# First MLP's output with its columns on partitions, mean squares by a ones matmul and Newton steps, two PSUM banks for the hidden layer

## The chip, the cores and the metric

One core of a Trainium2 chip (trn2) runs the whole program. The metric is the device time of one execution in microseconds, and less is better. Matmuls run on TensorE (PE in the profile, its weight loads PEld), elementwise work on VectorE (DVE), ScalarE (ACT) and GpSimd (POOL), and SyncE (SP) issues the DMAs. PSUM, where matmuls write, has eight banks in each partition; they are `ps[:, 0, :]` to `ps[:, 7, :]` here.

## The reference

Attention over 4 batches of 8 heads, 576 positions and 64 columns feeds two MLPs. All is in float32.

```python
# attention: softmax over means of 4 positions (144 of them), repeated 4 times,
# plus softmax over the positions nearer than 4
x = attn_out.transpose(0, 2, 1, 3).reshape(2304, 512)
h = x @ w_in                        # 512 -> 2048
y = (h * np.cos(h)) @ w_out         # 2048 -> 512, the first MLP's output
rms = np.sqrt(np.mean(y * y, axis=-1, keepdims=True) + 1e-06)
yn = y / rms * rms_g
g, val = yn @ w_gate, yn @ w_val    # 512 -> 1536
out = (g / (1 + np.exp(-g)) * val) @ w_out2
```

## The kernel before

**Numbers.** Every float32 operand of a large matmul is split into a high part (rounded to the matmul's format, a copy on ScalarE) and a low part (the rest, a subtraction on VectorE or GpSimd). `three` then adds three matmuls: low by high, high by low, high by high.

**First MLP.** The 2304 tokens are worked off in six passes (chunks c = 0 to 5) of 384 tokens. A pass has 16 hidden tiles f of 128 columns. In step f TensorE issues `up(f)`, twelve matmuls of 384 columns into bank `HB[f % NH]`, and then `down(f - 3)`, which adds the finished tile f - 3 into y; steps 16 to 18 have downs only, the last pass ends after step 15. Between up and down ScalarE and VectorE turn the tile into h cos h: turns (ScalarE, L751), reduction to one turn (VectorE, L1053 and L1055), Abs and Sin (ScalarE, L757 and L759), product with the bank (VectorE, L1061, `g_done`), high part (ScalarE, L686) and low part (VectorE, L972). L1061 is the last to read the bank. The wait `g_done, F1 * c + max(f + 1, NH)` ahead of up(f) asks for the product of tile f - NH of the same pass, or, for the first NH tiles, for all of the pass before.

`down_tile` takes three tiles of 128 tokens (t): the hidden tile is the stationary operand, the weights stream with 512 columns, so y has its tokens on partitions, in three banks. At a pass's end ScalarE squares the three tiles with a sum along the row (`squares`), VectorE copies them to `XY` (`copy_y`), and GpSimd takes the power -0.5 and multiplies (`scale_y`).

**Attention in the passes.** Passes 0 to 2 hold the attention of the next batch, four pairs of heads each. The tables `PE_WHERE` and `BESIDE_WHERE` set behind which step's up or down TensorE, and behind which tile's operation ScalarE and VectorE, do a piece of it. For pair 0 TensorE does the scores of the first head in step 1 behind up(1), those of the second in steps 2 and 3, and the two groups of transposes in step 4; VectorE and ScalarE do their parts between the operations of tiles 0 to 4. These passes are a loop on each engine, `Fori(0, ACH)` with ACH = 3; passes 3 and 4 are a second loop, pass 5 is written out.

**Second MLP.** It works in three blocks of 768 tokens (two passes' y each), 12 steps a block, i = 0 to 35. Its operands have columns on partitions. For that TensorE transposes y, four 128 by 128 at a time (`turn`, L1350), six times a block: in steps 5 to 10 of pass 5 for the first block, in steps 1 to 6 of the block before for the others. VectorE multiplies them by the gain out of PSUM (`turn_out`, L1006), then forms four sums (`operand_sum`) and the low parts (`operand_low`). A step has seven products (a Strassen-like scheme, two pairs of 384 columns give gate and value) in the banks CA and CB, `filler` puts the six tiles of the second down, 512 columns each, between them. In step 0 it puts the last three downs of the first MLP there instead. ScalarE copies CA out between products (`snapshot`, L806), VectorE adds CB (L1096, L1101, L1106).

**Weights of the second MLP** are split in passes 3 to 5 by ScalarE (`weight_high`) and GpSimd (`weight_low`, L578) through three buffers wp and stored by SyncE.

Lines in rows are those of this kernel: L1274 to L1276 the three matmuls of `three`, L1350 the transposes, L1055 and L1061 two operations of a hidden tile.

## Time and profile before

| what | value |
|---|---|
| median of 3 runs | 998.36 us (997.68 to 998.68) |
| the profiled execution | 998.75 us, its span 996.6 us |
| TensorE busy | 960.0 us (96%) |
| VectorE, ScalarE, GpSimd busy | 576.2, 502.7, 313.9 us |
| mean granted clock of TensorE | 0.993 |

The span runs from the first to the last instruction of the profiled execution. In rows of the timeline the first number is the start in us from the span's start, the second the duration in us; "x3" counts merged instructions; in brackets stands how long the engine was idle before, and what ended that. Matmuls overlap, so the distance from one start to the next tells their price and not their duration. A first matmul of a group of up has the form `ps<-xs,W`, of down `ps<-W,ring`, of a product `ps<-xo,wu`.

The six passes of the first MLP begin at about 56, 156, 256, 356, 422 and 489 us, the second MLP at 554 us.

### The profile page before, as it was taken

The page shows a single profiled execution, that of the slowest core. Times are in us where ns is not written, and L with a number is a line of the kernel's source. Part 1 is how long each engine was busy: PE and PEld are TensorE (multiplying, and loading weights), DVE is VectorE, ACT ScalarE, POOL GpSimd, SP SyncE. Part 2 cuts the span into 40 slices and gives each one's busy share as a digit, 9 for nine tenths or more (in the row PEclk, how much of TensorE's full clock was granted, in tenths as well). Part 3 has the DMA queues.
Part 4 walks back from the last instruction along what each step waited for, and adds up shares of the span by engine and source line. Part 5 has one row for each costly group of instructions (what it writes and reads, how often), then busy time and mean ns, then how long its engine had stood idle before and what let it go on. Part 6 is the DMA issues. An engine that isn't in the chain of part 4 may idle for free.

```text
span 996.6 us, 17754 instructions
## 1 busy us (share of the span) xinstructions
PE 960.0 (96%) x6104; PEld 852.7 (86%) x6104; DVE 576.2 (58%) x1225; ACT 502.7 (50%) x1081; POOL 313.9 (32%) x366
## 2 busy tenths in 40 slices
PE   7899998999899999999999899999999999999998
PEld 6677787888788889899988788899899999999997
DVE  6767766766676665564557544455744445544434
ACT  4456665666566667676666533333522224423322
POOL 5937862321232146568486112111300001000000
PEclk9999999999999999999999899999999999999999
DMA  9522110211021025434344575555565455575531
GB/s 305 192 95 93 54 52 25 80 55 52 26 80 53 22 76 185 164 147 169 126 170 149 210 253 149 154 152 161 149 217 151 149 161 166 153 229 158 160 106 64
DMA packets 66176, 132.35 MB, mean 133 GB/s; under 512 B 7088, under 2 KB 7216, under 8 KB 66096
## 3 DMA queue, kind: packets, MB, share of 16 engines
q1 hardware_dynamic: 66096, 131.27, 41.4%
q8 instruction: 52, 0.85, 0.4%
q14 instruction: 28, 0.23, 0.1%
HBM read 104.50 MB, written 26.74 MB: 132 GB/s over the span
## 4 chain that ended last, share of the span: by engine, by line
PE 75%; DVE 9%; ACT 7%; issue 4%; POOL 4%; DMA 1%; DVEq 0%; ACTq 0%; POOLq 0%; SPq 0%
PE ps L1274 23%; PE ps L1276 23%; PE ps L1275 23%; DVE ub L1055 2%; DVE ub L1053 2%; ACT ub L757 2%; PE ps L1193 2%; POOL W L521 2%; PE ps L1210 1%; ACT ub L759 1%; PE ps L1350 1%; DVE XY L893 1%; ACT ub L751 1%; DVE ub L1061 1%; ACT probd L626 1%
## 5 line engine op out<-in xcount | busy, mean ns | idle before, releaser
L1274 PE MATMUL ps<-xo,wu 128*128 128x384 f32 x504 | 169.5, 336 | 5.2 <-ACT gate_a L806 3.7
L1275 PE MATMUL ps<-xo,wu 128*128 128x384 f32 x504 | 170.5, 338 | 0.0
L1276 PE MATMUL ps<-xo,wu 128*128 128x384 f32 x504 | 170.0, 337 | 0.0
L1274 PE MATMUL ps<-xs,W 128*128 128x384 f32 x384 | 136.0, 354 | 0.9 <-DVE xs L968 0.9
L1276 PE MATMUL ps<-xs,W 128*128 128x384 f32 x384 | 131.7, 343 | 4.8 <-issue 4.8
L1275 PE MATMUL ps<-xs,W 128*128 128x384 f32 x384 | 131.3, 342 | 0.0
L1274 PE MATMUL ps<-W,ring 128*128 128x512 f32 x288 | 116.5, 405 | 0.0
L1276 PE MATMUL ps<-W,ring 128*128 128x512 f32 x288 | 113.5, 394 | 0.0
L1275 PE MATMUL ps<-W,ring 128*128 128x512 f32 x288 | 113.4, 394 | 0.0
L1274 PEld LDWEIGHTS ps<-xo,wu 128*128 128x128 f32 x504 | 95.3, 189 | 12.4 <-ACT gate_a L806 4.1
L1275 PEld LDWEIGHTS ps<-xo,wu 128*128 128x128 f32 x504 | 95.1, 189 | 6.7
L1061 DVE TENSOR_TENSOR ub<-ub,ps 128x384 f32<-128x384 f32 x96 | 53.0, 552 | 73.6 <-ACT ub L759 73.6
L1276 PEld LDWEIGHTS ps<-xo,wu 128*128 128x128 f32 x504 | 95.2, 189 | 0.0
L757 ACT ACTIVATE ub<-ub 128x384 f32<-128x384 f32 x96 | 50.4, 525 | 72.1 <-DVE ub L1055 72.1
L1276 PE MATMUL ps<-wo,ring 128*128 128x512 f32 x216 | 85.7, 397 | 0.0
L1275 PE MATMUL ps<-wo,ring 128*128 128x512 f32 x216 | 85.4, 395 | 0.0
L1274 PE MATMUL ps<-wo,ring 128*128 128x512 f32 x216 | 85.3, 395 | 0.1
L1274 PEld LDWEIGHTS ps<-xs,W 128*128 128x128 f32 x384 | 74.0, 193 | 12.2 <-issue 7.7
L1101 DVE TENSOR_TENSOR val_b<-val_b,ps 128x384 f32<-128x384 f32 x36 | 19.9, 554 | 100.7 <-ACT val_b L806 100.5
L1275 PEld LDWEIGHTS ps<-xs,W 128*128 128x128 f32 x384 | 74.1, 193 | 1.8
L1053 DVE TENSOR_SCALAR ub<-ub 128x384 f32<-128x384 f32 x96 | 46.8, 488 | 49.1 <-ACT ub L751 49.0
L1276 PEld LDWEIGHTS ps<-xs,W 128*128 128x128 f32 x384 | 73.9, 192 | 0.0
(134 smaller groups left out, 1852.3 us busy)
## 6 DMA issues: line engine op xcount, KB each, us to landing
wu<-wsplit SPq DMA_DIRECT2D x252, 256.0 KB, 2.8
wsplit<-wp SPq DMA_DIRECT2D x84, 256.0 KB, 2.0
W_raw<-w SPq DMA_DIRECT2D x8, 1024.0 KB, 15.1
qk<-qk SPq DMA_DIRECT2D x14, 576.0 KB, 4.0
gv<-wgv SPq DMA_DIRECT2D x12, 512.0 KB, 3.6
vw<-vwin SPq DMA_DIRECT2D x14, 384.0 KB, 3.2
out<-XY SPq DMA_DIRECT2D x18, 256.0 KB, 3.4
vg<-vgrp SPq DMA_DIRECT2D x26, 144.0 KB
```

Of the source, the lines that this page charges most:

```text
L521: g.tensor_tensor(lo, raw, hi.bitcast(F32), ALU.subtract).then_inc(unit_ready, 1)
L626: ins = a.activation(kind.probd[j][0:QT, s, t, :], kind.sd[s][:, t * SD:t * SD + SD], ACT.Exp, scale=SCALE_D, bias=dbias[0:QT, s, t:t + 1] ...
L751: a.activation(v, HB[f % NH], ACT.Identity, scale=INV_2PI, bias=consts[:, 0:1]).then_inc(turns_ready, 1)
L757: a.activation(v, v, ACT.Abs).then_inc(abs_ready, 1)
L1053: v.tensor_scalar(w, w, MAGIC, -2.0 * math.pi, ALU.subtract, ALU.mult).then_inc(angle0, 1)
L1055: v.tensor_tensor(w, w, HB[f % NH], ALU.add).then_inc(angle_ready, 1)
L1061: v.tensor_tensor(w, w, HB[f % NH], ALU.mult).then_inc(g_done, 1)
L1101: v.tensor_tensor(vb[:, :], vb[:, :], CB, ALU.add).then_inc(vb_ready, 1)
L1193: ins = t_.matmul(sl[64 * half:64 * half + 64, t * WIN:t * WIN + WIN], q[:, Q0[w]:Q0[w] + WIN], k[:, K0[w]:K0[w] + WIN], start=False, stop ...
L1274: t_.matmul(dst, a_lo, b_hi, start=first, stop=False, skip_group_check=True)
L1275: t_.matmul(dst, a_hi, b_lo, start=False, stop=False, skip_group_check=True)
L1276: return t_.matmul(dst, a_hi, b_hi, start=False, stop=last, skip_group_check=True)
```

## The change

**Layout.** `down_tile(f, k)` now takes four tiles of 128 columns of y: the weights are the stationary operand, the hidden tile streams with its 384 tokens. y comes out with columns on partitions, in four banks (2 to 5). `turn` and `turn_out` are gone, and so are the copies xa and xb: the operands are read from XY.

**Mean squares.** They are now sums over partitions. ScalarE and VectorE copy two tiles of y each. GpSimd squares and adds the four (`squares`) and splits the sum in two parts; TensorE multiplies these by a matrix of ones (`stats`, two matmuls); VectorE computes the inverse root by a guess from the bits and three Newton steps (`rms_step`, steps 0 to 3) and scales the four parts by it and the gain (steps 4 to 7). For y of passes 0 to 3 this happens in the pass behind; for the last two in the second MLP.

**Banks.** The hidden tiles have two banks (NH = 2), CA is bank 0 and CB bank 6, which attention also uses.

**Other.** Operand sums and low parts of the first block move to tiles 5 to 13 of pass 5, and VectorE does all its low parts; XON = 9 slots hold the seven operands so that the first two of the next block don't wait. Six buffers wp instead of three. TensorE and VectorE have pass 0 written out and loop over passes 1 and 2.

```diff
+WPN = 6
+XON = 9
+NEWTON = 3
+RMS_STEPS = 1 + NEWTON + KT
+GUESS = float(0x5F3759DF)
+STAT = 6
...
+    xt = at("xt", [P, 3, 2, CH], F32, slots_at)
+    xo = at("xo", [P, XON, 2, 2, CH], F32R, slots_at + 2 * 4096 + 1024)
...
-    X, Z = ps[:, 3, :], ps[:, 7, :]
-
-    NH = 3
+    X, Z = ps[:, 6, :], ps[:, 7, :]
+
+    NH = 2
     HB = [ps[:, i, 0:CH] for i in range(NH)]
-    YB = [ps[:, 4 + i, :] for i in range(TT)]
-
-    CA, CB = ps[:, 1, 0:CH], ps[:, 2, 0:CH]
-    Y2 = [ps[:, i, :] for i in (3, 7, 0, 4, 5, 6)]
-
-    def turn_bank(c, t):
-        return ps[:, 2, :] if c else ps[:, (3, 7)[t % 2], :]
+    YB = [ps[:, 2 + k, 0:CH] for k in range(KT)]
+    STATS = X[:, 0:CH]
+
+    CA, CB = ps[:, 0, 0:CH], ps[:, 6, 0:CH]
+    Y2 = [ps[:, i, :] for i in (7, 1, 2, 3, 4, 5)]
 
...
-    POOL_XO = (1, 3, 5)
-    XO_ORDER = ((0, 1, 3, 2, 4, 5, 6), (0, 1, 2, 3, 4, 5, 6))
+    XO_ORDER = ((0, 1, 6, 3, 2, 4, 5), (0, 1, 2, 3, 4, 5, 6), (0, 1, 2, 3, 4, 5, 6))
+    POOL_XO = ((), (1, 3, 5), (1, 3, 5))
+    DVE_XO = ((0, 1, 6, 3, 2, 4, 5), (0, 2, 4, 6), (0, 2, 4, 6))
...
-    TURN_F = 1
-    TURN_STEP = 5
+    SUM_F = 7
+    STAT_AT = ((1, 2, 3, 4, 5, 6, 7, 8), (8, 9, 10, 12, 13, 14, 15, 16))
...
-            scale_y(b - 1)
-
...
+        def squares(c):
+
+            def square(k, to):
+                if k < 2:
+                    hold(pool, y_copied, 2 * c + k + 1)
+                else:
+                    hold(pool, y_copied_act, 2 * c + k - 1)
+                return g.tensor_tensor(sq[:, to, :], y_part(c, k), y_part(c, k), ALU.mult)
+
+            if not (isinstance(c, int) and c == 0):
+                hold(pool, newton, (2 + 3 * NEWTON) * c)
+            square(0, 0).then_inc(sq_ready, 1)
+            for k in range(1, KT):
+                square(k, 1).then_inc(sq_ready, 1)
+                hold(pool, sq_ready, (2 * KT - 1) * c + 2 * k)
+                g.tensor_tensor(sq[:, 0, :], sq[:, 0, :], sq[:, 1, :], ALU.add).then_inc(sq_ready, 1)
+                hold(pool, sq_ready, (2 * KT - 1) * c + 2 * k + 1)
+            if not (isinstance(c, int) and c == 0):
+                hold(pool, stat_done, c)
+            g.tensor_tensor(sums_of_sq[:, 0, :], sq[:, 0, :], ones[:, 0:1].to_broadcast([P, CH]), ALU.mult).then_inc(sshi_ready, 1)
+            hold(pool, sshi_ready, c + 1)
+            g.tensor_tensor(sums_of_sq[:, 1, :], sq[:, 0, :], sums_of_sq[:, 0, :].bitcast(F32), ALU.subtract).then_inc(sslo_ready, 1)
+            hold(pool, sslo_ready, c + 1)
 
         batch(1, (5, 5, 5, 1))
         with pool.Fori(2, B) as b:
+            squares(b - 2)
             batch(b)
+        squares(ACH - 1)
+
...
+            if f == 3:
+                squares(ACH)
+            elif f == 8:
+                squares(ACH + 1)
...
+            for o in {8: (0,), 9: (1,), 10: (6,), 11: (3,), 12: (2, 4), 13: (5,)}.get(f, ()):
...
-        def squares(c):
-
-            for t in range(TT):
-                if t == 0:
-                    act.wait_ge(down_done, F1 * c + F1)
-                    act.wait_ge(rinv_ready, c + 1)
-                    act.wait_ge(glo_ready, F1 * c + F1)
-                else:
-                    act.wait_ge(ssq_ready, TT * c + t)
-                junk = ub[:, :, :].rearrange("p a n -> p (a n)")[:, 0:512]
-                a.activation(junk, YB[t], ACT.Square, accum_out=ssq[:, t:t + 1]).then_inc(ssq_ready, 1)
-            act.wait_ge(ssq_ready, TT * c + TT)
+        def copy_y(c):
+
+            act.wait_ge(down_done, F1 * c + F1)
+            for k in range(2, KT):
+                a.activation(y_part(c, k), YB[k], ACT.Copy).then_inc(y_copied_act, 1)
 
...
+        def rms_step(c, step, at_=STATS):
+
+            x, y, r = sq[:, 0, :], sq[:, 1, :], rms[:, :]
+            n = (2 + 3 * NEWTON) * c
+            if step == 0:
+                dve.wait_ge(stat_done, c + 1)
+                v.tensor_scalar(x, at_, 1.0 / DM, 1e-6, ALU.mult, ALU.add).then_inc(ms_ready, 1)
+                dve.wait_ge(ms_ready, c + 1)
+                v.tensor_scalar(r.bitcast(I32), x.bitcast(I32), -0.5, GUESS, ALU.mult, ALU.add).then_inc(newton, 1)
+                dve.wait_ge(newton, n + 1)
+                v.tensor_scalar(x, x, -0.5, None, ALU.mult).then_inc(newton, 1)
+            elif step <= NEWTON:
+                n += 2 + 3 * (step - 1)
+                dve.wait_ge(newton, n)
+                v.tensor_tensor(y, r, r, ALU.mult).then_inc(newton, 1)
+                dve.wait_ge(newton, n + 1)
+                v.tensor_tensor(y, y, x, ALU.mult).then_inc(newton, 1)
+                dve.wait_ge(newton, n + 2)
+                ins = v.scalar_tensor_tensor(r, y, 1.5, r, ALU.add, ALU.mult).then_inc(newton, 1)
+            else:
+                k = step - NEWTON - 1
+                if k == 0:
+                    dve.wait_ge(newton, n + 2 + 3 * NEWTON)
+                    dve.wait_ge(g_in, 16)
+                v.scalar_tensor_tensor(y_part(c, k), y_part(c, k), gcol[:, k:k + 1], r, ALU.mult, ALU.mult).then_inc(y_scaled, 1)
+
+        def operand_sum(c, step):
...
+            if 5 <= f <= 8:
+                operand_sum(0, f - 5)
+            for o in {9: (0,), 10: (1,), 11: (6,), 12: (3, 2), 13: (4, 5)}.get(f, ()):
+                operand_low(0, o)
...
+                if before and attention and f == 2:
+                    rms_step(c - 1, 0)
                 if attention:
                     attend(c, f, 1)
+                if before and not last and STAT + attention < f <= STAT + RMS_STEPS:
+                    rms_step(c - 1, f - STAT - 1)
...
-        with dve.Fori(0, ACH) as c:
+        hidden(0, True)
+        split_x(1)
+        copy_y(0)
...
+            for n, at_ in enumerate(STAT_AT):
+                if i in at_[1:]:
+                    rms_step(LASTC - 1 + n, at_.index(i))
...
+            if kind is Narrow and j == 0 and s == 0 and not (isinstance(b, int) and b == 1):
+                pe.wait_ge(ms_ready, b - 1)
...
-        def down_tile(f, t):
-            cols = slice(t * P, t * P + P)
+        def down_tile(f, k):
+            cols = slice(k * P, k * P + P)
             slot = 2 * f + 1
-            return three(YB[t], ring[:, f % 3, 0, cols], ring[:, f % 3, 1, cols], w_part(slot, 0), w_part(slot, 1), f == 0, f == F1 - 1)
+            return three(YB[k], w_part(slot, 0)[:, cols], w_part(slot, 1)[:, cols], ring[:, f % 3, 0, :], ring[:, f % 3, 1, :], f == 0, f == F1 - 1)
 
         def down(f):
-            for t in range(TT):
-                ins = down_tile(f, t)
+            for k in range(KT):
+                ins = down_tile(f, k)
             return ins
+
+        def stats(c, dst):
+
+            pe.wait_ge(sslo_ready, c + 1)
+            t_.matmul(dst, ones_r[:, :], sums_of_sq[:, 1, :], start=True, stop=False, skip_group_check=True)
+            t_.matmul(dst, ones_r[:, :], sums_of_sq[:, 0, :], start=False, stop=True, skip_group_check=True).then_inc(stat_done, 1)
 
         def attend(b, step, half):
 
...
-                        pe.wait_ge(y_copied, TT * c + TT)
+                    if f == 0 and before:
+                        pe.wait_ge(y_copied, 2 * c)
+                        pe.wait_ge(y_copied_act, 2 * c)
                     down(f).then_inc(down_done, 1)
-                if last and TURN_STEP <= step < TURN_STEP + PT6:
-                    turn(0, step - TURN_STEP)
+                if before and attention and step == 3:
+                    pe.wait_ge(diff_ready, 2 * PAIRS * (c + 1) + 2)
+                    stats(c - 1, STATS)
+                elif before and not attention and not last and step == STAT:
+                    stats(c - 1, STATS)
                 if attention:
                     attend(c + 1, step, 1)
...
-        with pe.Fori(0, ACH) as c:
+        chunk1(0, True)
+        with pe.Fori(1, ACH) as c:
             chunk1(c, True)
         with pe.Fori(ACH, LASTC) as c:
             chunk1(c, False)
-
-        def turn(c, t):
-
-            pe.wait_ge(y_scaled, PT6 * c + t + 1)
-            if c:
-                pe.wait_ge(gb_ready, F2 * (c - 1) + TURN_F + t + 1)
-            elif t >= 2:
-                pe.wait_ge(turned, t - 1)
-            bank, y = turn_bank(c, t), y2_tile(c, t)
-            for k in range(KT):
-                ins = t_.transpose(bank[:, k * P:k * P + P], y[:, k * P:k * P + P], ident[:, :])
-            ins.then_inc(tr_done, 1)
 
         def product(i, o, dst, first):
...
-                for n in ((0, 1), (2,), (3, 4), (5, 6), (7, 8))[slot]:
+                for n in ((0, 1, 2), (3,), (4, 5, 6), (7, 8, 9), (10, 11))[slot]:
...
-                pe.wait_ge(g_done, F1 * LASTC + F1 - 2 + NH)
+                pe.wait_ge(g_done, F1 * LASTC + F1 - 1 + NH)
             product(i, 0, CA, True)
             if i:
                 pe.wait_ge(gb_ready, i)
-            else:
-                pe.wait_ge(g_done, F1 * LASTC + F1 - 1 + NH)
-            if c < SC - 1 and TURN_F < f <= TURN_F + PT6:
-                pe.wait_ge(turned, PT6 * (c + 1) + f - TURN_F)
+            for n, at_ in enumerate(STAT_AT):
+                if i == at_[0] + 1:
+                    pe.wait_ge(ms_ready, LASTC + n)
...
-            if c < SC - 1 and TURN_F <= f < TURN_F + PT6:
-                turn(c + 1, f - TURN_F)
+            for n, at_ in enumerate(STAT_AT):
+                if i == at_[0]:
+                    pe.wait_ge(gb_ready, i + 1)
+                    stats(LASTC - 1 + n, CB)
```

TensorE, step 1 of the second MLP, around the place behind product 6 (`wo` with `ring_133` or `ring_134` is the second down). Before:

```order
L1276 MATMUL ps<-xo,wu_128 128x384
L1274 MATMUL ps<-wo,ring_133 128x512
L1275 MATMUL ps<-wo,ring_133 128x512
L1276 MATMUL ps<-wo,ring_133 128x512
L1350 MATMUL ps<-ident,XY 128x128 x4
L1274 MATMUL ps<-wo,ring_133 128x512
```

Now:

```order
L1306 MATMUL ps<-xo,wu_129 128x384
L1304 MATMUL ps<-wo,ring_134 128x512
L1305 MATMUL ps<-wo,ring_134 128x512
L1306 MATMUL ps<-wo,ring_134 128x512
L1330 MATMUL ps<-sums_of_sq,ones_r 128x384
L1331 MATMUL ps<-sums_of_sq,ones_r 128x384
L1304 MATMUL ps<-wo,ring_134 128x512
```

The four transposes are gone here and in steps 2 to 6; two ones matmuls stand in step 1 and again in step 8.

VectorE, attention passes, tile 2 and the copy of the transposed probabilities behind it. Before:

```order
L1053 TENSOR_SCALAR ub<-ub 128x384
L1055 TENSOR_TENSOR ub<-ub,ps 128x384
L972 TENSOR_TENSOR ring<-ub,ring 128x384
L1061 TENSOR_TENSOR ub<-ub,ps 128x384
L1052 REGISTER_ALU
```

Now, in passes 1 and 2:

```order
L1070 TENSOR_SCALAR ub<-ub 128x384
L1072 TENSOR_TENSOR ub<-ub,ps 128x384
L982 TENSOR_TENSOR ring<-ub,ring 128x384
L1078 TENSOR_TENSOR ub<-ub,ps 128x384
L1009 TENSOR_SCALAR sq<-ps 128x384
L1011 TENSOR_SCALAR rms<-sq 128x384
L1012 ISA
L1013 TENSOR_SCALAR sq<-sq 128x384
L953 COPY probd_85<-ps 72x288
```

The first step of the inverse root comes between the product of tile 2 and what follows it.

VectorE, pass 5 of the first MLP, from what stands behind tile 13 to the start of tile 15 (each tile begins with the reduction of `ub`). Before:

```order
L1020 TENSOR_TENSOR xb<-xb 128x768
L1023 TENSOR_TENSOR xt<-xa,xt 128x768
L1053 TENSOR_SCALAR ub<-ub 128x384
L1055 TENSOR_TENSOR ub<-ub,ps 128x384
L972 TENSOR_TENSOR ring<-ub,ring 128x384
L1061 TENSOR_TENSOR ub<-ub,ps 128x384
L1028 TENSOR_TENSOR xo<-xt,xo 128x768
L1028 TENSOR_TENSOR xo<-xb,xo 128x768
L1053 TENSOR_SCALAR ub<-ub 128x384
```

Now:

```order
L1052 TENSOR_TENSOR xo<-XY,xo 128x768
L1052 TENSOR_TENSOR xo<-xt,xo 128x768
L1070 TENSOR_SCALAR ub<-ub 128x384
L1072 TENSOR_TENSOR ub<-ub,ps 128x384
L982 TENSOR_TENSOR ring<-ub,ring 128x384
L1078 TENSOR_TENSOR ub<-ub,ps 128x384
L1070 TENSOR_SCALAR ub<-ub 128x384
```

The sums that stood behind tile 13 come earlier now, the low parts that stood behind tile 14 stand behind tile 13 at the latest, and between tiles 14 and 15 VectorE does nothing else.

## Rows read from the trace of the kernel before

**Rows 1.** The page, part 4: the chain that ended last, by engine.
```profile
PE 75%; DVE 9%; ACT 7%; issue 4%; POOL 4%; DMA 1%; DVEq 0%; ACTq 0%; POOLq 0%; SPq 0%
```

**Rows 2.** Busy time: stretch, length, each engine's busy us, clock, DMA.
```profile
157.00:257.00 100.00, 95.51 (x800) 80.53 (x800) 66.70 (x175) 62.69 (x136) 25.62 (x37) 0.98 0.17 53
356.00:422.00 66.00, 66.00 (x334) 59.92 (x333) 37.06 (x71) 46.12 (x103) 40.86 (x50) 1.00 0.40 146
```

**Rows 3.** Timeline: start, duration, instruction; TensorE and VectorE, start of pass 4.
```profile
426.61 0.33 PE L1274 MATMUL ps<-xs,W 128*128 128x384 f32 x1
...
427.69 0.56 DVE L1061 TENSOR_TENSOR ub<-ub,ps 128x384 f32<-128x384 f32 x1 [1.24 <-ACT ub L759]
...
428.69 0.33 PE L1274 MATMUL ps<-xs,W 128*128 128x384 f32 x1
...
430.96 0.55 DVE L1061 TENSOR_TENSOR ub<-ub,ps 128x384 f32<-128x384 f32 x1 [0.77 <-ACT ub L759]
...
432.85 0.33 PE L1274 MATMUL ps<-xs,W 128*128 128x384 f32 x1
```

**Rows 4.** Timeline, TensorE and VectorE, in attention pass 1.
```profile
159.30 0.33 PE L1276 MATMUL ps<-xs,W 128*128 128x384 f32 x1 [2.57 <-issue]
...
166.34 0.45 PE L1274 MATMUL ps<-xs,W 128*128 128x384 f32 x1
...
167.72 0.54 DVE L1061 TENSOR_TENSOR ub<-ub,ps 128x384 f32<-128x384 f32 x1
...
169.51 0.44 PE L1274 MATMUL ps<-xs,W 128*128 128x384 f32 x1
...
175.43 0.33 PE L1274 MATMUL ps<-xs,W 128*128 128x384 f32 x1
...
179.73 0.56 DVE L1061 TENSOR_TENSOR ub<-ub,ps 128x384 f32<-128x384 f32 x1 [2.05 <-ACT ub L759]
...
181.37 0.42 PE L1274 MATMUL ps<-xs,W 128*128 128x384 f32 x1
...
200.56 0.42 PE L1274 MATMUL ps<-xs,W 128*128 128x384 f32 x1
...
201.51 0.55 DVE L1061 TENSOR_TENSOR ub<-ub,ps 128x384 f32<-128x384 f32 x1 [2.05 <-ACT ub L759]
```

**Rows 5.** Busy time of two stretches; the granted clock is the 0.50.
```profile
161.00:164.00 3.00, 3.00 (x11) 3.00 (x11) 1.41 (x2) 0.89 (x2) 2.73 (x4) 0.50 0.03 5
560.20:566.80 6.60, 5.07 (x15) 4.88 (x16) 2.99 (x5) 3.82 (x6) 0.00 (x0) 0.50 0.01 2
```

**Rows 6.** Timeline: TensorE's first matmul of steps 6, 7 and 8, second MLP.
```profile
635.56 0.34 PE L1274 MATMUL ps<-xo,wu 128*128 128x384 f32 x1
...
647.82 0.34 PE L1274 MATMUL ps<-xo,wu 128*128 128x384 f32 x1
...
659.34 0.33 PE L1274 MATMUL ps<-xo,wu 128*128 128x384 f32 x1
```

**Rows 7.** Timeline, TensorE, in pass 5 of the first MLP.
```profile
503.82 0.33 PE L1274 MATMUL ps<-xs,W 128*128 128x384 f32 x1
...
523.75 0.30 PE L1350 MATMUL ps<-ident,XY 128*128 128x128 f32 x1 [1.71 <-DVE xa L1006]
...
533.37 0.42 PE L1274 MATMUL ps<-xs,W 128*128 128x384 f32 x1
```

**Rows 8.** Timeline, TensorE, from the first MLP's end into the second.
```profile
550.18 0.33 PE L1274 MATMUL ps<-xs,W 128*128 128x384 f32 x1
...
561.73 0.69 PE L1274 MATMUL ps<-xo,wu 128*128 128x384 f32 x1 [3.71 <-ACT gate_a L806]
...
574.26 0.33 PE L1274 MATMUL ps<-xo,wu 128*128 128x384 f32 x1
```

**Rows 9.** Groups of instructions: line, shapes, count, busy and mean, idle ahead.
```profile
L1101 DVE TENSOR_TENSOR val_b<-val_b,ps 128x384 f32<-128x384 f32 x36 | 19.9, 554 | 100.7 <-ACT val_b L806 100.5
...
L578 POOL TENSOR_TENSOR wp<-gv,wp 128x256 fp32r<-128x256 f32 x48 | 39.0, 813 | 32.3 <-ACT wp L722 29.6
```

243 lines of the change are left out of this document (99 added, 144 removed).

## The prediction

> **What bounds the kernel now.** First I read the chain that ended last, on the profile's page [rows 1]: TensorE carries 75% of it, VectorE 9%, ScalarE 7%. Then the busy time of two stretches [rows 2]. In a layer pass without attention TensorE is busy 66.00 of 66 us; in one with attention 95.5 of 100, VectorE 67, ScalarE 63, GpSimd 26. So whatever TensorE no longer issues is time won, and whatever makes it wait for VectorE or ScalarE is time lost. VectorE and ScalarE work as one serial chain per hidden tile f: turns (L751), reduction (L1053, L1055), Abs, Sin, product (L1061). I call the product's end *free(f)*: from then on the bank of HB that up(f) filled may be written again. The sum below is made against the profiled execution, 998.75 us (span 996.6 and 2.1 around it); the median of the runs is 998.36.
>
> **Two banks instead of three.** With NH = 3, up(f) waits for free(f-3); with NH = 2 for free(f-2). Where up(f+2) starts before free(f) today, the new wait costs at least the difference. In the pass that begins at 422 us [rows 3], up(2) starts at 426.61 and free(0) is 427.69 + 0.56 = 428.25; up(3) starts at 428.69 and free(1) is 430.96 + 0.55 = 431.51. Up(2) waits 1.6 us; behind its own 2.08 us up(3) waits again until free(1), 2.8 after its start today. ScalarE no longer squares y there, which brings this forward by some 0.2: 2.6 a pass. Nothing stands behind the waiting matmuls that could fill in, since the first down comes in step 3; down(0) and all later work move back. Later in a pass up and down together take 4.16 us a step [rows 3], the chain has two of these for a tile, and I count nothing. Passes 3, 4 and 5: 2.3 + 2.6 + 2.6 = +7.5.
>
> In the attention passes VectorE and ScalarE put softmax work of the next batch between two tiles. In pass 1 [rows 4] up(2) starts at 166.34, free(0) is 168.26; worse, up(4) starts at 175.43 and free(2) is 179.73 + 0.56 = 180.29. These 12.0 us from free(0) to free(2) belong to ScalarE and VectorE (two softmax halves and a table load), so TensorE can't shorten them; that it delivers local and downsampled scores later adds an estimated 0.4. Shift at up(4): 4.9 + 0.4 = 5.3; in passes 0 and 2 I read the same. +15.9 for three. Lower end: 4.9 each, 14.7.
>
> Right behind it stands a dependency that three banks hid: ScalarE and VectorE, after free(2), copy the first transposed probabilities, which TensorE makes behind up(4). Today up(4) is long done by then; now both engines wait until up(4) and seven transposes have run (some 3.7 us), then need 0.5 for the copy and some 3.4 for tile 3 (free(1) follows free(0) by 3.3 in rows 3), so free(3) is about 7.6 after up(4) starts, while TensorE would reach up(5) after 5.9 (its pitch today, 175.43 to 181.37 [rows 4]). +1.6 a pass, between 0 and 2.5: +4.8. In step 6 the same figure as at f=2 recurs smaller [rows 4]: up(8) starts at 200.56, free(6) is 202.06; +1.5 a pass, +4.5.
>
> **The clock.** After 2.57 us of idle at 156.7 [rows 4] the granted clock was 0.50 in 161 to 164 [rows 5]; after 3.71 us before 561.73 [rows 8] it was 0.50 from 560.2 to 566.8. Half clock for 3.4 us costs 1.7, for 6.6 us 3.3, less what falls into idle time (about a third in the second case). The new idle before up(4) is about 4 us long, in each attention pass. I take 2.2 each, +6.6; bounds 0 and 3.3 each. In the other three passes the idle comes in two pieces of 1.6 and 1 us, both shorter than the shortest above that was followed by half clock: 0, upper end 1.7 each.
>
> **The loop over the attention passes begins at 1.** TensorE's program now has pass 0 written out, so the jump back happens once, not twice. At the jump to pass 1 it idles for 2.57 us with "issue" as the reason [rows 4] and then has the half-clock stretch [rows 5], together 2.57 + 1.8 = 4.4. Taken as gone: -4.4. Bounds: the straight code may be fetched late as well (0), or all goes.
>
> **Transposes out.** Steps of the second MLP with four transposes take 647.82 - 635.56 = 12.26 us, without 659.34 - 647.82 = 11.52 [rows 6]; twelve such steps, 0.75 each: -9.0. In the last pass of the first MLP six more: from 503.82 to 533.37 six steps take 29.55 instead of 6 x 4.16 = 25.0, one with 1.71 of idle [rows 7]: -4.6. VectorE's multiplications out of the turned banks go too; they lay beside matmuls.
>
> **The ones matmuls.** Six pairs at 384 columns, by up's twelve in 2.08 us 0.17 each, 0.35 a pair. Two lie in passes 1 and 2 within the new idle time, four count: +1.4. They wait for GpSimd: 9 operations of 384 columns a pass, of which the row for 256 columns shows 0.81 us [rows 9]; by columns 1.2 each, 11 us behind the copy of y, between 7 and 15. They are asked for in step 3 of an attention pass (over 15 us after its start) and step 6 otherwise (over 21): hidden. GpSimd's own queue behind it is value sums and the splitting of gate and value weights; six wp buffers instead of three let ScalarE run ahead meanwhile.
>
> **Newton steps.** On VectorE each is three operations that wait for each other, 0.55 apiece by the nearest row, 1.7 a step. In the second MLP VectorE is idle 100.7 us in 36 steps ahead of L1101, 2.8 a step [rows 9]: hidden. In passes 3 and 4 the chain grows to some 4.6 us a step for four steps, 1.7 in all against about 2.7 of lead: hidden. In passes 1 and 2 the second falls directly ahead of L1053 of tile 10, right behind a softmax: between 0 and 1.7, I take 1.1: +2.2.
>
> **Down in four tiles.** Up and down take 4.16 a step, so nine matmuls of 512 columns take 2.08 [rows 3], just what twelve of 384 take in up: 0, between -1 and +2 in all 96.
>
> **The handover to the second MLP.** Up(15) starts at 550.18, product 2 of step 0 at 561.73 after 3.71 us of idle, at half clock; step 1 begins at 574.26, 24.1 us after up(15) [rows 8]. The operand sums and low parts are moved from steps 11 to 14 into 5 to 13, so tiles 14 and 15 run clean: I get free(15) at 7 us after up(15) starts, the snapshot at 8.1, with TensorE there at 7.9. Then up(15) and down(12) 4.2, the seven products 7.4 (11.52 less six tiles of 0.69) and twelve down tiles 6.3, with 0.4 of waits: 18.3. -5.8; bounds -2.3 (still waits, half clock stays) and -6.3.
>
> **Sum.** 7.5 + 15.9 + 4.8 + 4.5 + 6.6 + 1.4 + 2.2 = 42.9 lost; 4.4 + 9.0 + 4.6 + 5.8 = 23.8 won; +19.1. Some of TensorE's own small waits in the attention passes (about 2 us each) should shrink when it runs later; I take 2 off for all: +17, 1016 us against 998.75.
>
> A page of the Trainium skill speaks for the other side: TensorE: Matmul & The Clock Gate, "HAM oscillation — how this bites in real kernels", reports a kernel in which doubling PSUM buffers on top of a good loop order gave no further gain, that is, bank depth need not matter. By that rule the 32.7 us that hang on the bank, and the clock behind it, would be nothing. The rows agree with it only for the steady steps of a pass; at its start they don't.
>
> **Rivals.** *Two banks are enough* (faster): if VectorE and ScalarE caught up because their own work shrinks at a pass's start (no squares, fewer copies), the bank terms and the clock (39.3) vanish, 998.4 - 23.8 + 3.6 gives 978. Against it: 12 us between free(0) and free(2) hold no square and no copy of y. It decides from free(2) coming before 176. *The waits are there but alone*: no coupling behind up(4), no half clock, Newton hidden, TensorE's own waits shrink more: 19.1 - 4.8 - 6.6 - 2.2 - 3 = +3, 1001 to 1005. For it: every term is read from starts in a schedule that will shift. *The clock takes more*: half clock for 6.6 us in all three attention passes and 3.4 in the others, and the handover keeps its idle: 3.3 + 5.1 + 3.5 more, 1028. *The change doesn't reach the chip's order*: the wait counts are formed from NH everywhere, so no chance worth a number.
>
> **Numbers.** Forecast 0.65 (1008 to 1024), two banks enough 0.09, the waits alone 0.15, the clock takes more 0.11. The range reaches from 1001 to 1029. What this measurement can tell from no change is about 0.2%, 2 us: faster 0.09, within it 0.04 (the lower edge of the waits alone), slower 0.87.
>
> **What would show it.** In the profile after: idle of TensorE that ends on VectorE's product ahead of up matmuls, 1.6 and 1 us at the start of passes 3 to 5, about 4 us before the fifth up of passes 0 to 2; half clock behind the latter; no idle with "issue" at the first pass's end; second MLP steps of 11.5 us throughout, and step 0 near 14 instead of 19.9. If the first three passes are not longer than 100 us each, the forecast is wrong in its main term; if step 0 is still near 20, in the handover.

## The result and the profile after

| kernel | median of its runs | range |
|---|---|---|
| before | 998.02 us (4 runs) | 996.59 to 998.68 |
| after | 1034.89 us (4 runs) | 1033.68 to 1037.66 |

The ratio is 1.0375 (95% interval 1.0350 to 1.0399): 3.75% slower. The forecast was 1016 with a range of 1001 to 1029. It had the sign, and the time lies 6 us above the range. The profiled execution of after has a span of 1032.7 us against 996.6, so 36.1 us are to be explained where 17 were forecast.

Part 1 of the page of after:

```profile
PE 961.7 (93%) x6332; PEld 889.6 (86%) x6332; DVE 630.7 (61%) x1300; ACT 495.9 (48%) x1057; POOL 336.4 (33%) x385
```

TensorE is as busy as before (960.0) and stands still 34 us longer; VectorE has 54.5 us more work. The chain that ended last, which answers to [rows 1]:

```profile
PE 70%; DVE 13%; ACT 7%; POOL 5%; issue 4%; DMA 0%; POOLq 0%; ACTq 0%; DVEq 0%; SPq 0%
```

VectorE's share of the chain went from 9% to 13%. The groups of instructions say what TensorE waits for (behind the bar: busy time, mean ns, idle before and its releaser):

```profile
L1304 PE MATMUL ps<-xs,W 128*128 128x384 f32 x384 | 139.3, 363 | 48.1 <-DVE ub L1078 46.6
```

46.6 us in front of an up matmul end on VectorE's product L1078, the instruction that frees a bank; before, the same matmuls waited 0.9. Busy time by pass of after, as in [rows 2]:

```profile
165.00:274.00 109.00, 97.48 (x855) 88.21 (x854) 75.94 (x192) 62.48 (x134) 29.51 (x41) 0.98 0.16 49
381.00:456.00 75.00, 69.05 (x390) 67.03 (x389) 52.58 (x86) 44.73 (x99) 44.70 (x53) 1.00 0.36 131
```

In pass 3 VectorE was busy for 37.06 of 66 us and is now for 52.58 of 75. To see where the time went I take the distance between the first up matmuls of neighbouring passes, in us; the last column runs from the first product to the end.

| kernel | pass 0 | 1 | 2 | 3 | 4 | 5 | second MLP |
|---|---|---|---|---|---|---|---|
| before | 102.0 | 100.2 | 99.3 | 66.8 | 66.8 | 65.2 | 442.3 |
| after | 109.9 | 108.4 | 108.0 | 74.6 | 76.5 | 71.7 | 428.3 |
| difference | +7.9 | +8.2 | +8.6 | +7.8 | +9.7 | +6.5 | -14.0 |

With 1.3 us more ahead of pass 0 that is the 36 us. The terms of the prediction, sorted by pass, give about 27.6 for passes 0 to 2, 2.7, 3.0 and -2.0 for passes 3, 4 and 5, and -14.1 for the second MLP. The attention passes together came out within 3 us of the forecast and the second MLP within 0.1 us, and **the miss is in passes 3 to 5: 24.0 instead of 3.6.** That the attention passes fit is in part luck: two errors of opposite sign meet there, as the part on the prediction shows.

What was foreseen is there. At the start of pass 3 up(2) and up(3) wait, in attention pass 1 up(4) and up(5) do; these timelines of TensorE answer to [rows 3] and [rows 4]:

```profile
388.01 0.45 PE L1304 MATMUL ps<-xs,W 128*128 128x384 f32 x1 [2.04 <-DVE ub L1078]
...
390.90 0.44 PE L1304 MATMUL ps<-xs,W 128*128 128x384 f32 x1 [0.51 <-DVE ub L1078]
```

```profile
172.64 0.44 PE L1304 MATMUL ps<-xs,W 128*128 128x384 f32 x1 [1.50 <-DVE ub L1078]
...
184.94 0.68 PE L1304 MATMUL ps<-xs,W 128*128 128x384 f32 x1 [3.49 <-DVE ub L1078]
...
185.74 0.52 PE L1306 MATMUL ps<-xs,W 128*128 128x384 f32 x1
...
193.28 0.44 PE L1304 MATMUL ps<-xs,W 128*128 128x384 f32 x1 [1.10 <-DVE ub L1078]
```

Durations of 0.52 instead of 0.33 behind 184.94 are half clock. Windows of 3.4 to 3.7 us that begin at the end of three waits (columns as in [rows 2]; the clock is the third number from the end):

```profile
65.60:69.00 3.40, 3.40 (x11) 3.40 (x12) 1.69 (x4) 3.00 (x5) 0.00 (x0) 0.51 0.00 0
184.90:188.30 3.40, 3.36 (x11) 3.36 (x12) 1.52 (x3) 0.00 (x0) 1.92 (x3) 0.51 0.02 7
193.30:197.00 3.70, 3.70 (x60) 3.25 (x60) 3.33 (x6) 1.75 (x4) 0.00 (x0) 1.00 0.00 0
```

Half clock followed waits of 1.60 and 3.49 us, not the one of 1.10. The first products of steps 0, 1, 2 and 3 of the second MLP, in answer to [rows 6] and [rows 8], are 13.66, 12.14 and 11.53 us apart; the forecast was 14 and 11.5, against 19.9 for step 0 before. Step 1, with two ones matmuls, takes 0.6 more than a step without:

```profile
604.38 0.44 PE L1304 MATMUL ps<-xo,wu 128*128 128x384 f32 x1
...
618.04 0.33 PE L1304 MATMUL ps<-xo,wu 128*128 128x384 f32 x1
...
630.18 0.34 PE L1304 MATMUL ps<-xo,wu 128*128 128x384 f32 x1
...
641.71 0.33 PE L1304 MATMUL ps<-xo,wu 128*128 128x384 f32 x1
```

Two things were not foreseen. **Late in passes 3 and 4** up(12) and up(13) wait:

```profile
430.29 0.45 PE L1304 MATMUL ps<-xs,W 128*128 128x384 f32 x1 [1.32 <-DVE ub L1078]
...
435.99 0.44 PE L1304 MATMUL ps<-xs,W 128*128 128x384 f32 x1 [1.26 <-DVE ub L1078]
```

VectorE shows why. Here is its timeline for one tile, from one L1078 (the product that frees the bank) to the next:

```profile
417.74 0.55 DVE L1078 TENSOR_TENSOR ub<-ub,ps 128x384 f32<-128x384 f32 x1 [0.77 <-ACT ub L779]
418.21 1.10 DVE L1017 TENSOR_TENSOR sq<-rms 128x384 f32<-128x384 f32 x1
419.35 0.97 DVE L1019 TENSOR_TENSOR sq<-sq 128x384 f32<-128x384 f32 x1
420.36 0.98 DVE L1021 SCALAR_TENSOR_TENSOR rms<-sq,rms 128x384 f32<-128x384 f32 x1
421.26 0.35 DVE L1070 TENSOR_SCALAR ub<-ub 128x384 f32<-128x384 f32 x1
421.65 0.56 DVE L1072 TENSOR_TENSOR ub<-ub,ps 128x384 f32<-128x384 f32 x1
422.12 0.55 DVE L982 TENSOR_TENSOR ring<-ub,ring 128x384 fp32r<-128x384 f32 x1
423.44 0.55 DVE L1078 TENSOR_TENSOR ub<-ub,ps 128x384 f32<-128x384 f32 x1 [0.78 <-ACT ub L779]
```

The tile takes 5.70 us, TensorE's up and down 4.16; the products of tiles 9, 10 and 11 come 5.70, 6.24 and 5.70 us behind the one before. The Newton step in it (L1017 to L1021) takes 3.05 us, not the 1.7 of the prediction. The next rows, of pass 4, show on what that depends; those of GpSimd in the same time stand below them:

```profile
500.62 1.11 DVE L1017 TENSOR_TENSOR sq<-rms 128x384 f32<-128x384 f32 x1
501.76 0.98 DVE L1019 TENSOR_TENSOR sq<-sq 128x384 f32<-128x384 f32 x1
502.77 0.56 DVE L1021 SCALAR_TENSOR_TENSOR rms<-sq,rms 128x384 f32<-128x384 f32 x1
```

```profile
500.56 0.75 POOL L609 TENSOR_TENSOR wp_more<-gvs,wp_more 128x256 fp32r<-128x256 f32 x1 [2.94 <-ACT wp_more L751]
501.39 0.93 POOL L609 TENSOR_TENSOR wp_more<-gv,wp_more 128x256 fp32r<-128x256 f32 x1
```

GpSimd ends at 502.32. The operation that begins after that takes 0.56, those beside it 1.0 to 1.1. The ones with an operand in PSUM (L1078, L1072) take 0.55 either way. L1021 at 502.77 and the L1070 and L982 of the tile above, without an operand in PSUM, take their short time because GpSimd is idle then. **In pass 5** up(6) stands still for 5.64 us and runs at half clock behind it. ScalarE had stood still ahead of it, for GpSimd's sums:

```profile
552.60 0.42 ACT L751 ACTIVATE wp<-gvs 128x256 fp32r<-128x256 f32 x1 [5.06 <-POOL gvs L595]
555.83 0.42 ACT L751 ACTIVATE wp<-gvs 128x256 fp32r<-128x256 f32 x1 [2.82 <-POOL gvs L599]
556.16 0.56 ACT L771 ACTIVATE ub<-ps,consts 128x384 f32<-128x384 f32 x1
```

L771 forms the turns of the next tile, its first operation. GpSimd's queue in the same time, its last squares and the first sum behind them:

```profile
548.70 1.00 POOL L575 TENSOR_TENSOR sq<-sq 128x384 f32<-128x384 f32 x1
549.78 0.83 POOL L579 TENSOR_TENSOR sums_of_sq<-sq,ones 128x384 fp32r<-128x384 f32 x1
550.68 1.01 POOL L581 TENSOR_TENSOR sums_of_sq<-sq,sums_of_sq 128x384 fp32r<-128x384 f32 x1
551.77 0.73 POOL L595 TENSOR_TENSOR gvs<-gv 128x256 f32<-128x256 f32 x1
```

### The profile page after: what moved, and what is told of

It is laid out like the page before. It is cut to its first block, busy times and chain, and to the rows that moved or that the text cites. A ratio compares the mean times of both kernels' runs of the same rounds, so it can differ in the third digit from the quotient of the medians.

```text
span 1032.7 us, 18242 instructions
## 1 busy us (share of the span) xinstructions
PE 961.7 (93%) x6332; PEld 889.6 (86%) x6332; DVE 630.7 (61%) x1300; ACT 495.9 (48%) x1057; POOL 336.4 (33%) x385
## 4 chain that ended last, share of the span: by engine, by line
PE 70%; DVE 13%; ACT 7%; POOL 5%; issue 4%; DMA 0%; POOLq 0%; ACTq 0%; DVEq 0%; SPq 0%
PE ps L1304 22%; PE ps L1306 21%; PE ps L1305 21%; DVE ub L1070 3%; DVE ub L1072 2%; ACT ub L779 2%; ACT ub L777 2%; PE ps L1221 2%; POOL W L538 1%; DVE ub L1078 1%; PE ps L1238 1%; PE ps L1281 1%; DVE sq L1019 1%; DVE sq L1017 1%; ACT L779 1%
## 5 line engine op out<-in xcount | busy, mean ns | idle before, releaser
L1304 PE MATMUL ps<-xs,W 128*128 128x384 f32 x384 | 139.3, 363 | 48.1 <-DVE ub L1078 46.6
L1306 PE MATMUL ps<-xs,W 128*128 128x384 f32 x384 | 133.6, 348 | 0.0
L1305 PE MATMUL ps<-xs,W 128*128 128x384 f32 x384 | 133.3, 347 | 0.0
L1304 PE MATMUL ps<-ring,W 128*128 128x384 f32 x384 | 132.4, 345 | 0.8 <-DVE ring L982 0.8
L1306 PE MATMUL ps<-ring,W 128*128 128x384 f32 x384 | 128.7, 335 | 0.0
L1305 PE MATMUL ps<-ring,W 128*128 128x384 f32 x384 | 128.5, 335 | 0.0
L1304 PEld LDWEIGHTS ps<-xs,W 128*128 128x128 f32 x384 | 75.4, 196 | 59.2 <-DVE ub L1078 34.7
L1078 DVE TENSOR_TENSOR ub<-ub,ps 128x384 f32<-128x384 f32 x96 | 53.0, 552 | 74.1 <-ACT ub L779 74.1
L1070 DVE TENSOR_SCALAR ub<-ub 128x384 f32<-128x384 f32 x96 | 55.5, 579 | 37.2 <-ACT ub L771 37.2
L1304 PEld LDWEIGHTS ps<-ring,W 128*128 128x128 f32 x384 | 72.3, 188 | 4.8 <-issue 4.1
L1305 PEld LDWEIGHTS ps<-xs,W 128*128 128x128 f32 x384 | 75.9, 198 | 0.0
L1306 PEld LDWEIGHTS ps<-xs,W 128*128 128x128 f32 x384 | 75.7, 197 | 0.0
```

The source lines that it names most:

```text
L1070: v.tensor_scalar(w, w, MAGIC, -2.0 * math.pi, ALU.subtract, ALU.mult).then_inc(angle0, 1)
L1078: v.tensor_tensor(w, w, HB[f % NH], ALU.mult).then_inc(g_done, 1)
L1304: t_.matmul(dst, a_lo, b_hi, start=first, stop=False, skip_group_check=True)
L1305: t_.matmul(dst, a_hi, b_lo, start=False, stop=False, skip_group_check=True)
L1306: return t_.matmul(dst, a_hi, b_hi, start=False, stop=last, skip_group_check=True)
```

## Experiments

Each kernel is held against before by its ratio on the same chip; after has 1.0375. Spans and pass times are those of one profiled execution each. Before itself had medians of 998.0, 995.1, 997.0 and 996.1 us on the chips used, so a difference of spans can be off by some 3 us, and the ratio decides on the total. "Not told apart" below means that the 95% intervals of two ratios overlap. Narrow stands for Newton operations on 8 columns.

**1. Before with two banks.** The handover's waits follow the banks. All else stays: down in three tiles of 512 columns, the transposes and the squares on ScalarE.

```diff
-    NH = 3
+    NH = 2
-    CA, CB = ps[:, 1, 0:CH], ps[:, 2, 0:CH]
-    Y2 = [ps[:, i, :] for i in (3, 7, 0, 4, 5, 6)]
+    CA, CB = ps[:, 0, 0:CH], ps[:, 2, 0:CH]
+    Y2 = [ps[:, i, :] for i in (3, 7, 1, 4, 5, 6)]
```

> The kernel before with NH = 2 alone (CA in bank 0 and one output tile in bank 1, so that the handover stays legal); layout, transposes, squares and weights as before. Theory (the second waits on the bank are the largest part of the loss): passes 0 to 2 grow by 7 to 9 us each, clock included, passes 3 to 5 by 2.3 to 2.8 each, together +28 to +34, about 1029 us. TensorE idles 3.5 to 4 us ahead of the fifth up of passes 0 to 2. Rival (the new work on VectorE and GpSimd is what makes the engines late, the bank only passes it on): under +10.

Measured: ratio 1.0309 (1.0291 to 1.0328), which is 30.8 us. Passes 111.6, 107.9, 107.4, 69.5, 69.8, 66.7, that is +9.7, +7.7, +8.1, +2.7, +3.0, +1.6. The theory holds, with passes 0 and 4 above its ranges and pass 5 below. The waits at the start of pass 3 and before up(4) and up(5) of pass 1 are close to those of after:

```profile
388.74 0.44 PE L1274 MATMUL ps<-xs,W 128*128 128x384 f32 x1 [1.66 <-DVE ub L1061]
```

```profile
191.05 0.69 PE L1274 MATMUL ps<-xs,W 128*128 128x384 f32 x1 [3.86 <-DVE ub L1061]
...
200.21 0.44 PE L1274 MATMUL ps<-xs,W 128*128 128x384 f32 x1 [0.68 <-DVE ub L1061]
```

Two banks alone cost about 3.1%. In the attention passes of this profile that is 25.5 us; after has 24.7 there, with Newton's cost and the loop's gain in it. The 25.5 may be some us too high: the profiled execution took 1031.6 us, 5.0 above the median of its runs, and its span grew by 33.2 where the ratio says 30.8. In passes 3 to 5 it is 7.3 us (forecast 7.5) of after's 24.0, and 16.7 are left.

**2. Before with pass 0 of the attention passes written out,** so that TensorE loops over passes 1 and 2 as in after.

```diff
-        with pe.Fori(0, ACH) as c:
+        chunk1(0, True)
+        with pe.Fori(1, ACH) as c:
             chunk1(c, True)
```

> The kernel before, TensorE's loop over attention passes from 1, pass 0 written out, nothing else. Theory (the idle with reason issue is the jump back): the 2.57 us of idle and the half clock behind it at the first pass's end go, -3.5 to -4.5 us, about 994. Rival (the idle is caused by something else at a pass's start, such as the copy of y): no change, 998.

Measured: ratio 0.9961 (0.9947 to 0.9975), passes 0 to 2 100.2, 96.7, 96.9. By the ratio that is 3.9 us less; the theory holds in the total. Yet both stretches of idle time that nothing released are gone, that between passes 1 and 2 too, although a jump back stands there still, and pass 0, which has no turn ahead of it, shows 1.7 less too. The up group that had 4.8 us of it:

```profile
L1276 PE MATMUL ps<-xs,W 128*128 128x384 f32 x384 | 130.0, 339 | 0.0
```

**3. Before with all three attention passes written out.**

```diff
-        with pe.Fori(0, ACH) as c:
+        for c in range(ACH):
             chunk1(c, True)
```

> The before kernel with TensorE's three attention passes written out one after the other instead of as a loop of three. With only pass 0 written out the ratio was 0.9961 (0.9947 to 0.9975) and both stretches of idle time that nothing released (2.57 and 2.26 us) were gone, the second one too although a loop of two with a jump back stayed. Theory (the idle time goes with a long loop body whose code comes back from far, and is gone as soon as the loop is short of one turn): the same as with pass 0 alone, 0.9950 to 0.9972. Rival (the jump back still costs something that the profile shows in another row, such as the wait of 1.7 us for the exponents at the start of passes 1 and 2): 0.990 to 0.994.

Measured: ratio 0.9969 (0.9957 to 0.9981), the same as pass 0 alone. The theory holds; the second jump costs nothing that can be measured. Either is faster than both kernels of this case.

**4. After with GpSimd's squares of the fourth panel (y of pass 4) behind the last of the second MLP's twelve weight tiles** instead of behind the ninth. The f of this piece of GpSimd's program counts weight tiles, not hidden tiles; in the trace the squares begin at 587.15 instead of in front of up(6).

```diff
-            elif f == 8:
+            elif f == F2 - 1:
                 squares(ACH + 1)
```

> The changed kernel, GpSimd's squares of y of pass 4 moved behind the last weight (from behind f = 8). Theory (in pass 5 ScalarE waits 5.1 and 2.8 us for gate sums that stand behind the squares in GpSimd's queue, the product of tile 4 is late, up(6) idles 5.6 us and the clock falls): pass 5 shrinks from 71.7 to 64 to 66 us, total -6 to -8, about 1028. Rival (ScalarE would wait for free wp buffers or stores anyway): -2 at most.

Measured: ratio 1.0374 (1.0354 to 1.0393), no gain in the time where the theory had 6 to 8 us. Pass 5 took 67.5 instead of 71.7 us (theory 64 to 66); its up(6) is now without a wait, and up(15) has a new one:

```profile
559.95 0.33 PE L1304 MATMUL ps<-xs,W 128*128 128x384 f32 x1
...
596.10 0.41 PE L1304 MATMUL ps<-xs,W 128*128 128x384 f32 x1 [1.88 <-DVE ub L1078]
```

So the cause of the 5.64 us is shown, and moving it is worth 4.2 in its pass. In this profile passes 2 and 3 took 1.4 and 0.8 us more, with half clock in other places; the span fell by 2.8, the median relative to before not at all. The gain is seen in its pass and is not shown in the total.

**5. After with the Newton steps of passes 3 and 4 on a PSUM operand** (y in the free bank Z), so that two of the three operations have one input in PSUM, with GpSimd as busy as ever.

```diff
-            x, y, r = sq[:, 0, :], sq[:, 1, :], rms[:, :]
+            x, y, r = sq[:, 0, :], sq[:, 1, :] if y is None else y, rms[:, :]
...
-                    rms_step(c - 1, f - STAT - 1)
+                    rms_step(c - 1, f - STAT - 1, y=None if attention else Z[:, 0:CH])
```

> The changed kernel, in passes 3 and 4 the Newton steps' intermediate y lies in PSUM bank 7, which is free there, instead of SBUF. Theory (VectorE operations with two SBUF inputs take 1.1 instead of 0.55 us while GpSimd works): the second and third operation of a Newton step fall from 0.98 to 0.55 us in those passes, the first stays at 1.09; passes 3 and 4 shrink by 1.5 to 2.5 us each, -3 to -5 in all. Rival (the operations are long because they wait for each other's results): durations and time stay.

Measured: ratio 1.0363 (1.0339 to 1.0388); passes 3 and 4 72.8 and 74.1, 1.8 and 2.4 less, within the theory's 1.5 to 2.5 each. Passes 1 and 2 of this profile took 0.3 and 1.0 more, and the total is not told apart from after's. The same step in its timeline of VectorE:

```profile
419.71 0.56 DVE L1078 TENSOR_TENSOR ub<-ub,ps 128x384 f32<-128x384 f32 x1 [0.77 <-ACT ub L779]
420.18 1.11 DVE L1017 TENSOR_TENSOR ps<-rms 128x384 f32<-128x384 f32 x1
421.32 0.57 DVE L1019 TENSOR_TENSOR ps<-ps,sq 128x384 f32<-128x384 f32 x1
421.93 0.56 DVE L1021 SCALAR_TENSOR_TENSOR rms<-ps,rms 128x384 f32<-128x384 f32 x1
...
424.74 0.56 DVE L1078 TENSOR_TENSOR ub<-ub,ps 128x384 f32<-128x384 f32 x1 [0.77 <-ACT ub L779]
```

Only L1017, whose two inputs are still in SBUF, takes 1.11; the other two fell from 0.98 to 0.57 and the tile from 5.70 to 5.03 us. That shows the contention with GpSimd as the cause of the long operations.

**6. After with the Newton operations on 8 of 384 columns.** The other 376 columns keep the starting value of the inverse root, so the kernel leaves their Newton steps out.

```diff
             elif step <= NEWTON:
+                x, y, r = sq[:, 0, 0:8], sq[:, 1, 0:8], rms[:, 0:8]
```

> The changed kernel with VectorE's two operations of each Newton step on 8 of the 384 columns: the inverse root is left at its starting value for the other columns, all else is as in the changed kernel. It takes away VectorE's time for the steps (3.05 us for one step in passes 3 and 4) and keeps their place and number. Theory (the steps make VectorE's work for a tile 5.7 us where TensorE's is 4.16, three tiles in a row in each pass that has them): the idle stretches before up(12) and up(13) of passes 1 to 4 go, and the late down behind; 2 to 3 us from each of passes 1 and 2, 4 to 5 from passes 3 and 4; in all 12 to 15 us less, a ratio to before of 1.023 to 1.026. Rival (what is late there is the chain of the mean squares, or GpSimd's sums, and not VectorE's time): under 5 us less, as with the steps on a PSUM operand, ratio 1.033 or more.

Measured: ratio 1.0268 (1.0231 to 1.0305), span 1020.9, 11.8 less (10.7 by the ratio). Passes 1 to 4 took 105.8, 105.4, 70.8, 72.9: 2.6, 2.5, 3.8 and 3.5 less, and the waits before up(12) and up(13) are gone. The mechanism of the theory holds; its sizes were too high: 12 to 15 us in all and 4 to 5 in passes 3 and 4 each. The tile is now 4.10 us:

```profile
417.61 0.56 DVE L1079 TENSOR_TENSOR ub<-ub,ps 128x384 f32<-128x384 f32 x1 [0.78 <-ACT ub L779]
418.08 0.70 DVE L1018 TENSOR_TENSOR sq<-rms 128x8 f32<-128x8 f32 x1
418.81 0.17 DVE L1020 TENSOR_TENSOR sq<-sq 128x8 f32<-128x8 f32 x1
419.01 0.59 DVE L1022 SCALAR_TENSOR_TENSOR rms<-sq,rms 128x8 f32<-128x8 f32 x1
...
421.71 0.56 DVE L1079 TENSOR_TENSOR ub<-ub,ps 128x384 f32<-128x384 f32 x1 [0.77 <-ACT ub L779]
```

**7. After with three banks in passes 3 to 5.**

```diff
+    HB3 = [Z[:, 0:CH], HB[0], HB[1]]
+    def hb(f, attention):
+        return HB[f % NH] if attention else HB3[f % 3]
...
-                    pe.wait_ge(g_done, F1 * c + max(f + 1, NH))
+                    pe.wait_ge(g_done, F1 * c + max(f + attention, NH))
```

> The changed kernel with three banks for the inner layer again in passes 3 to 5 (the bank that holds Z or the mean squares in the attention passes is free there), two banks in passes 0 to 2. The before kernel with two banks took 2.7, 3.0 and 1.6 us more in passes 3 to 5 than before; the changed one 7.8, 9.7 and 6.5 more. Theory (a third bank is one step of 4.16 us of slack for whatever makes the end of a tile late: the Newton steps on VectorE and the sums on GpSimd): the idle stretches before up(2) and up(3) go, those before up(12) and up(13) of passes 3 and 4 (1.3 us each in the records, and the late down behind them) shrink to near nothing, the 5.6 us before up(6) of pass 5 to about 1.5; passes 3, 4 and 5 take 68 to 70, 68 to 70 and 67 to 68 us instead of 74.6, 76.5 and 71.7; in all 15 to 20 us less than the changed kernel, a ratio to before of 1.018 to 1.023. Rival (the third bank pays only for the waits at the start of each pass, and the engines behind are late whatever the banks): 7.3 us less, ratio 1.030.

Measured: ratio 1.0369 (1.0343 to 1.0396). Passes 3 to 5 73.1, 76.2, 68.5, second MLP 433.0. My theory fell, and the rival too. The waits at the start of the passes are gone and those before up(12) and up(13) as well; the one before up(6) of pass 5 is now one of 5.13 before a down. In pass 3 waits come back before the downs:

```profile
445.99 0.41 PE L1309 MATMUL ps<-ring,W 128*128 128x384 f32 x1 [1.86 <-DVE ring L987]
...
450.18 0.41 PE L1309 MATMUL ps<-ring,W 128*128 128x384 f32 x1 [1.87 <-DVE ring L987]
```

A third bank lets one late tile pass. It doesn't help where VectorE needs more time per tile than TensorE over several tiles and has too little to spare before the pass ends. What pass 5 gains the second MLP loses: its step 0 takes 4.7 us more (2.97 of idle for ScalarE's snapshot, and half clock), as it does, by 6, in experiments 8, 10 and 11. VectorE's product of tile 15 ends 74.3 us after the start of pass 5 in after and 74.3 here. TensorE is through with its ups sooner and then waits for the same product and the snapshot behind it. From the start of pass 5 to the end of the kernel it is 501.5 us here and 500.0 in after.

**8. Three banks and narrow Newton steps together** (the edits of 7 and 6).

> The changed kernel with three banks in passes 3 to 5 and with VectorE's two operations of each Newton step on 8 of the 384 columns (the inverse root stays at its starting value for the others). The three banks alone brought nothing in the sum: passes 3, 4, 5 took 73.1, 76.2, 68.5 us instead of 74.6, 76.5, 71.7 while the second MLP took 4.7 us more, and the idle time moved from the ups to the downs at the end of passes 3 and 4. The narrow steps alone made passes 3 and 4 70.8 and 72.9. Theory (VectorE has more work than TensorE over tiles 11 to 15, and a bank only puts off when that shows; with the work gone the bank is worth what it is in the before kernel, 2.7 to 3.0 us a pass): passes 3 and 4 at 67 to 68 and 68.5 to 70 us; ratio to before 1.019 to 1.023 (narrow steps alone 1.0268). Rival (the third bank is worth nothing here whatever VectorE does, since the sums of squares on GpSimd and the longer VectorE operations beside them set the starts): passes 3 and 4 at 70 and 72 or more, ratio 1.026 or more.

Measured: ratio 1.0219 (1.0196 to 1.0243), passes 3 and 4 67.2 and 69.7. The theory holds, the rival (1.026 or more) doesn't: once VectorE keeps up, the third bank is worth 3.7 and 3.2 us a pass.

**9. After with the first transposes of pass 0 ahead of up(4).**

```diff
+    PE_WHERE0 = (((1, 0), (2, 0), (3, 0), (3, 1), (4, 1), (5, 0)),) + PE_WHERE[1:]
-            for what, j in steps_at(PE_STEPS, PE_WHERE, (step, half)):
+            for what, j in steps_at(PE_STEPS, PE_WHERE0 if isinstance(b, int) and b == 1 else PE_WHERE, (step, half)):
```

> The changed kernel with TensorE's transposes of the first head of a pair, in pass 0 only, ahead of up(4) instead of behind it. Theory (with two banks up(4) waits 3.9 us for VectorE's last operation on tile 2, the transposes stand behind it in TensorE's queue, and what copies them and the next tile's end come late for that: the 2.0 us before up(5)): the wait before up(4) stays near 3.9, that before up(5) falls from 2.0 to under 0.7, pass 0 takes 1.3 to 2 us less, ratio 1.0355 to 1.036. Rival (up(5) waits for the second bank alone, and what is behind it is slack): within 0.5 us of the changed kernel, ratio 1.037 to 1.0375; or the copies that now come earlier push VectorE's last operation on tile 2 back, and up(4) waits longer: 1 us more, 1.0385.

Measured: ratio 1.0355 (1.0330 to 1.0379), pass 0 107.5, 2.4 less, and no wait before up(5). So the coupling is real: the copies, and with them the next tile, wait for the transposes that stand behind up(4). The total is not told apart from after's; pass 2 of this profile took 3.3 more, with half clock there.

**10. Three banks, late squares and early transposes.**

> The changed kernel with three edits together: three banks in passes 3 to 5, GpSimd's squares of the fourth panel behind the last tile of pass 5 instead of behind tile 8, and the early transposes in pass 0. Theory (each takes its own wait): passes 3 to 5 at 68 to 70, 68 to 70 and 65 to 66 us, pass 0 1.5 us shorter; 17 to 24 us less than the changed kernel, ratio 1.014 to 1.020; still slower than before, since the two banks in the attention passes stay (the before kernel with two banks took 9.7, 7.7 and 8.1 us more in these). Rival (the edits pay for the same waits): no more than the three banks alone, within 1 us.

Measured: ratio 1.0282 (1.0256 to 1.0308), span 1023.4: 9.3 us less than after, not 17 to 24, since passes 3 and 4 stayed at 73.2 and 74.6 and the second MLP took 434.3. Pass 5 took 62.2: with both edits the waits before its ups are gone and one of 1.56 before a down is left, where either edit alone left 67.5 or more. But from the start of pass 5 to the end the kernel takes 496.4 us, and 495.7 with the late squares alone: behind tile 15 the third bank gives nothing.

**11. All four edits** (10 and the narrow steps).

> The changed kernel with all four: three banks in passes 3 to 5, the narrow Newton steps (inverse root left at its starting value in 376 of 384 columns), GpSimd's squares of the fourth panel behind pass 5, and the early transposes in pass 0. It is the closure of the account: what is left should be the two banks of the attention passes (7.7 to 9.7 us a pass by the before kernel with two banks, less what the early transposes and the loop from 1 give) and the second MLP's gain. Theory: pass 0 105 to 106, passes 1 and 2 105 to 107 each, pass 3 67 to 68, pass 4 68.5 to 70, pass 5 62 to 63, second MLP 432 to 435; span 1003 to 1008, ratio 1.008 to 1.014. Rival (the edits overlap and there is a cost not yet named in passes 3 to 5): span 1013 or more, ratio 1.018 or more.

Measured: span 1003.8, ratio 1.0148 (1.0125 to 1.0171). Passes 104.4, 105.8, 105.4, 67.2, 69.7, 62.1, second MLP 434.4. The span and all stretches but pass 0 (0.6 below) are in the theory's ranges, the ratio is 0.0008 above its own. This profiled execution was the fastest of its four, 4.1 us below their median, at a clock of 0.992 against 0.986 to 0.990, so its pass times may flatter the kernel by up to as much. Within that the account closes: what is left against before in passes 3 to 5 is 0.3 us, in the attention passes 14.2, in the second MLP -7.9 instead of -14.0. The 6 us between these last two are pass 5's lateness, which the third bank moves into step 0.

## Why the prediction was wrong

**The step that failed is "Newton steps", where it says of passes 3 and 4: "the chain grows to some 4.6 us a step for four steps, 1.7 in all against about 2.7 of lead: hidden."** Each operation was priced at 0.55 us by the nearest row. The row shown is L1101 [rows 9], which has an operand in PSUM and stands in the second MLP, where GpSimd is idle. In passes 3 and 4 GpSimd works beside the Newton operations, and they take 0.97 to 1.11. The products of three tiles come 5.70, 6.24 and 5.70 us apart, not 4.6: 5.2 us late in all, against a lead of 2.7 in the forecast and 2.2 in the trace (up(10) comes 8.3 behind up(8), free(8) 6.1). The 3 us left over are about what up(12) and up(13) wait, 2.6. Measured by experiment 6: 3.8 and 3.5 us instead of 0. The trace of before had a fitting row, two inputs in SBUF beside GpSimd at the end of pass 3:

```profile
418.90 1.05 DVE L968 TENSOR_TENSOR xs<-XY,xs 128x384 fp32r<-128x384 f32 x1
```

The Trainium skill states the mechanism (SBUF — State Buffer, "SBUF: two separate sides"): a VectorE operation with two inputs in SBUF and a GpSimd operation that reads SBUF take one port pair in turn, and whichever comes second is blocked for the whole instruction. The rows agree (0.56 alone, 0.97 to 1.11 beside GpSimd, 0.57 with a PSUM operand). That the contention and not the Newton steps' own work breaks the forecast is argued from these durations: at 0.55 an operation a tile takes an estimated 4.3 us (5.70 less 3.05 plus 1.65), 0.4 late in three, well within the lead. No run has the steps in full and GpSimd idle; experiment 5, which shortens two of the three, gives 1.8 and 2.4 us back. In passes 1 and 2 the term was 1.1 apiece and measured 2.6 and 2.5. Over the four passes Newton cost 12.4 us where 2.2 were forecast.

**The second is in "The ones matmuls": "six wp buffers instead of three let ScalarE run ahead meanwhile".** I asked whether the sums of squares come in time for TensorE, and they do. I didn't ask who waits for what stands behind nine operations in GpSimd's queue. ScalarE does, for 5.06 us, and it can't reach L771, with which the next tile begins: 5.64 us before up(6) and half clock. By experiment 4 it is worth 4.2 us in pass 5.

**Left of passes 3 to 5.** Of 20.4 us missing these two are 11.5. Another part is probably the same contention in other operations. Before up(2) and up(3) of pass 4 TensorE waited 2.07 and 1.61 us, where GpSimd squares the last panel, and VectorE's reduction beside it, which has one input, also in SBUF, takes 1.06 instead of 0.36:

```profile
459.12 1.06 DVE L1070 TENSOR_SCALAR ub<-ub 128x384 f32<-128x384 f32 x1 [1.56 <-ACT ub L771]
```

By subtraction (after, less before with two banks, less the narrow steps' gain) passes 3 and 4 hold 1.3 and 3.1 us of such. No run took them away by itself. Pass 5 holds some 4 more. The forecast let its last tiles "run clean", but with the operand sums and low parts between the tiles VectorE is again slower than TensorE: in experiment 4 the products of tiles 6 to 12 come 4.6 us apart and those of 13 and 14 6.3 and 5.6, and up(15) waits for it. No run took this away: from the start of pass 5 to the end before took 507.4 us, the forecast was 16.1 less, that is 491.3, and no kernel came under the 495.7 of experiment 4. That VectorE's work there is the cause is argued and not shown.

**Two banks: right in mechanism, too high in the attention passes.** Start of passes 3 to 5: 7.5 forecast, 7.3 measured. In the attention passes the bank, the coupling (the copies that wait for the transposes behind up(4)), step 6 and the clock were 31.8 together, and experiment 1 has 25.5, which may be some us too high. In pass 0 of after, up(4) came 5.4 later (5.3 forecast) and up(5) 3.1 more (1.6 forecast); at up(8) the pass was 9.5 behind, and by up(10) 1.6 of it was given back, out of TensorE's own waits. So the terms at the fifth and sixth up were not too high but, for the coupling, too low; what was too high is their sum over a pass. This excess and Newton's 2.9 us too little in passes 1 and 2 cancel in part, and that is the luck in the attention passes.

**Clock.** By one minus the mean clock, times the span, half clock took at most 6.8 us of before and 14.2 of after. The statement that waits of 1.6 us are too short for it was wrong: the stretch from 65.60 shows 0.51 behind 1.60 us of idle.

**Loop from 1.** Forecast -4.4; experiment 2 has -0.39% of the time, 3.9 us. The size is right, the step only in part: it took away the idle time of one turn of two and called it the jump back. Both went, the second with its jump still there, and in before the 2.57 us stand behind the first two matmuls of pass 1 and not ahead of the pass. So a turn was priced too high, and what makes the idle time is open.

**Transposes out, handover, down in four tiles.** Second MLP -14.1 forecast, -14.0 measured: step 0 is 6.2 shorter (5.8 forecast), the twelve steps with transposes 0.75 each, the two with ones matmuls 0.6 longer (0.35 forecast). The pitch of up and down stayed at 4.16. Right. The 4.6 us for the six transposes of pass 5 can't be told from what else changed there; by the tiles of 4.6 us that VectorE sets in their place, part of it did not come.

**The rival from the Trainium skill** (TensorE: Matmul & The Clock Gate, "HAM oscillation — how this bites in real kernels"). Its case, in which doubling PSUM buffers gave no further gain, would have made the bank's terms zero here. Experiment 1 decides against it for this kernel: a third bank is worth 3.1%.

## What to carry to other kernels

Price an operation from a row in which the same neighbours work, or bound it by the dearest row of its kind; for VectorE the question here was whether an operation has an operand in PSUM (0.55 us either way) or only operands in SBUF while GpSimd works (up to twice as long). When an engine gets more work, compare its time per tile with the period of the bottleneck: under it, a lead or a buffer hides the work, above it every tile adds to the delay, and another buffer only moves the wait. Of work that is put into a queue, ask who waits for what is queued behind it.

## What the runs showed that was not expected

- The slowing of VectorE is waiting, not bandwidth: an operation on 8 columns in experiment 6 took 0.70 us at 418.08, until an operation of GpSimd ended at 418.75, and the next 0.17 at 418.81. GpSimd is slowed in its turn: its 128x256 operations take 0.73 alone and up to 1.34 beside VectorE.
- A loop of three passes had 2.57 and 2.26 us of idle without a releaser at its turns; a loop of two with the first pass ahead of it has none at its single turn, and the kernel takes 0.39% less time.
- Half clock followed one wait of 1.60 us and not another of 2.07 (462.62 to 465 ran in full clock), and its place shifts between kernels that differ little: pass 2 took 1.4 us more in experiment 4 and 3.3 more in experiment 9, neither of which changes that pass.
